# ACT's queue issues the first output-gate loads once both gate rows have landed

## What is computed

```python
for t in range(S):
    m_new = maximum(f_gate[:, :, t] + m, i_gate[:, :, t])
    f_stab, i_stab = exp(f_gate[:, :, t] + m - m_new), exp(i_gate[:, :, t] - m_new)
    m = m_new
    C = f_stab * C + i_stab * einsum('bhd,bhe->bhde', vt, kt)
    n = f_stab * n + i_stab * kt
    denom = maximum(abs(n . qt), 1.0)
    y[:, :, t] = sigmoid(o_gate[:, :, t]) * (C @ qt) / denom
x = y as (B, S, 320)
u = x + (relu(x^T @ w_tok1) @ w_tok2)^T
out = u + relu(u @ w_ch1) @ w_ch2
```

## Time and profile before

| | us |
|---|---|
| median of three runs | 469.45 (467.89 to 469.51) |
| time of the profiled execution | 467.59 |
| its span from the first to the last instruction | 465.9 |
| PE busy in the span | 442.2 (95%) |
| DVE busy | 264.2 |
| ACT busy | 228.9 |
| POOL busy | 176.8 |

### The profile page before, as it was taken

How to read it: one execution, slowest core, us unless ns; L and a number is a source line. 1 busy time by engine, 2 the same in 40 slices (tenths; PEclk the granted TensorE clock), 3 DMA queues, 4 the chain that set the end, 5 groups by cost and what they waited for, 6 DMA issues and landing times.

```text
span 465.9 us, 9523 instructions
## 1 busy us (share of the span) xinstructions
PE 442.2 (95%) x3471; PEld 408.0 (88%) x3471; DVE 264.2 (57%) x592; ACT 228.9 (49%) x570; POOL 176.8 (38%) x239
## 2 busy tenths in 40 slices
PE   6999989699999998999999998999999998999996
PEld 2577978589999997899999997899999997999996
DVE  6889964677766537666675227466685325222212
ACT  4665447657666247766653227966663113211111
POOL 6625410567665232676662203466663000000000
PEclk9999999999999999999999999999999999999999
DMA  7556990143444412444454012444410010000101
GB/s 210 195 156 185 348 267 30 37 123 118 138 135 153 135 46 86 138 139 138 127 161 127 13 42 85 135 128 137 139 59 1 2 42 1 0 2 0 44 1 42
DMA packets 36520, 47.38 MB, mean 102 GB/s; under 512 B 3324, under 2 KB 28986, under 8 KB 36474
## 3 DMA queue, kind: packets, MB, share of 16 engines
q1 hardware_dynamic: 35674, 45.79, 32.3%
q10 hardware_dynamic: 800, 0.98, 0.7%
HBM read 42.73 MB, written 4.03 MB: 100 GB/s over the span
## 4 chain that ended last, share of the span: by engine, by line
PE 80%; ACT 7%; DVE 5%; issue 4%; DMA 2%; SPq 1%; POOL 0%; DVEq 0%; ACTq 0%
PE pC L1155 31%; PE pA L1226 6%; PE pA L1227 6%; PE pA L1228 6%; PE pS L1067 6%; PE pA L1155 4%; PE pY L1124 4%; PE pA L1231 3%; PE pA L1230 3%; PE pY L1103 2%; PE pN L1079 2%; ACT gb L608 1%; PE pA L1185 1%; DMA u<-i_gate_dram 1%; DMA qz<-qT_dram 1%
## 5 line engine op out<-in xcount | busy, mean ns | idle before, releaser
L976 DVE SCALAR_TENSOR_TENSOR h_lo<-pA,h_hi 128x384 fp32r<-128x384 f32 x96 | 53.3, 555 | 133.1 <-ACT h_hi L758 133.1
L758 ACT ACTIVATE h_hi<-pA 128x384 fp32r<-128x384 f32 x96 | 46.7, 486 | 127.2 <-PE pA L1231 127.2
L1155 PE MATMUL pC<-wc_hi,h_hi 128*128 128x320 f32 x288 | 94.1, 327 | 0.8 <-DVE wc_lo L843 0.7
L1155 PE MATMUL pC<-wc_lo,h_hi 128*128 128x320 f32 x288 | 88.7, 308 | 0.0
L1155 PE MATMUL pC<-wc_hi,h_lo 128*128 128x320 f32 x288 | 88.4, 307 | 0.0
L490 POOL TENSOR_TENSOR gb<-gb,pb 128x384 f32<-128x384 f32 (+1 forms) x54 | 48.2, 893 | 81.9 <-ACT pb L618 81.9
L1226 PE MATMUL pA<-uT_hi,wc_hi 128*128 128x384 f32 x192 | 65.2, 340 | 1.9 <-DVE uT_hi L954 1.9
L1227 PE MATMUL pA<-uT_lo,wc_hi 128*128 128x384 f32 x192 | 64.7, 337 | 0.0
L1228 PE MATMUL pA<-uT_hi,wc_lo 128*128 128x384 f32 x192 | 64.4, 335 | 0.0
L1155 PEld LDWEIGHTS pC<-wc_hi,h_hi 128*128 128x128 f32 x288 | 54.0, 188 | 2.1 <-DVE h_lo L976 1.0
L1155 PEld LDWEIGHTS pC<-wc_lo,h_hi 128*128 128x128 f32 x288 | 54.2, 188 | 0.1
(11 more groups left out here) (128 smaller groups left out, 882.1 us busy)
## 6 DMA issues: line engine op xcount, KB each, us to landing
gb<-g_dram SPq DMA_DIRECT2D x18, 512.0 KB, 3.9
kv<-kvN_dram SPq DMA_DIRECT2D x24, 324.0 KB, 3.5
kd<-kT_dram SPq DMA_DIRECT2D x24, 180.0 KB
qz<-qT_dram SPq DMA_DIRECT2D x72, 60.0 KB
out_dram<-u SPq DMA_DIRECT2D x24, 160.0 KB, 1.9
qd<-qT_dram SPq DMA_DIRECT2D x20, 180.0 KB, 2.6
gq<-g_dram SPq DMA_DIRECT2D x45, 60.0 KB
wc_raw<-w_ch_dram SPq DMA_DIRECT2D x6, 384.0 KB, 5.3
```

The costliest lines, as they stand in the source:

```text
L758: nc.scalar.activation(h2[0][:, slot % 2], pA[slot % 2][:, 0:HALF], ACT.Relu).then_inc(h2_hi, 1)
L976: nc.vector.scalar_tensor_tensor(h2[1][:, slot % 2], pA[slot % 2][:, 0:HALF], 0.0, h2[0][:, slot % 2].bitcast(F32), ALU.max, ALU.subtract) ...
L1155: ins = mm(dst, a[p], b[q], start=first and n == 0, stop=last and n == 2)
```

## The change

ACT waits until both gate transfers have landed (`gates_in` at 32, the condition on which DVE's first scan waits too) before it issues its two loads of the first output gate. Nothing is removed and no transfer changes its size or its queue.

```diff
             o_tiles = o_gate[0, :, :].rearrange("(c p) d -> p c d", p=L)
+            act.wait_ge(gates_in, 32)
             for i, (first, last) in enumerate(O_PARTS):
                 act.dma_start(x[:, first:last], o_tiles[:, first:last]).then_inc(o_in[i], 16)
             sigmoid(0)
```

## The result

| | before | changed |
|---|---|---|
| median of six runs, us | 469.21 (467.89 to 469.51) | 472.62 (471.52 to 473.24) |
| profiled execution, us | 467.59 | 473.20 |
| span, us | 465.9 | 471.5 |

The changed kernel is slower: ratio 1.0077, 95% interval 1.0059 to 1.0094, that is 3.4 us. The forecast was +1.7, with a range that held the time; the sign was right and the size half. One execution of the changed kernel on the second chip took 1751.82 us, and nothing here shows why; no figure in this text counts it.

The account below looks back on a forecast made before the run. It took PE's nearly unbroken run from the query decays at 15.65 as the bound. Landing +2.6, waits -0.25 and -0.19, POOL slack -0.5 gave +1.7: 469.3 us profiled, 471.1 by the median; range 468.5 to 473.8.

Parts of the forecast that it names:

- The wait and the gates: Start of the kernel: the wait costs ACT at most 0.1 us; input gates land at 4.15, winning DVE 1.9 us.
- The third rival: Input gates still land near 6.1 because DMA engines are starting up; about +3.7 us; chance 0.07.
- The landing of the output gate: ACT's two loads, issued at about 4.2, land at 9.5, 2.6 us later than before, with ends 1.8 and 3.4.
- ACT's strand: On ACT, a fixed 4.79 us from landing to the end of `wT`; the 0.25 wait behind it goes.
- PE's gap and the clock: PE idles 3 to 4 us before spreading step 2 at about 15.2; whether its clock falls there was left open.
- The rival with a chance of 0.22: PE's clock falls in the new gap before step 2's spread, costing 1.8 more: about +3.5 us; chance 0.22.
- PE's wait for DVE: Before the query decays, PE's 0.19 us wait for DVE goes, since DVE's strand is done at 13.7.
- What is swallowed after: At segment 2's transposes, PE's 0.5 us wait for POOL absorbs part of the 2.16 shift, leaving +1.7.
- The rest of the chain moves along: After those transposes, later PE, DVE and SP steps shift with PE, at no cost and no gain.
- The sum: Whole kernel: +1.7 us, with a shift of 0.9 to 2.5 for the ends of the landing; chance 0.56.

Follow-up runs that it names:

- the repeat: The changed kernel itself run again, nothing edited, on a second chip: 471.87, 473.20 and 474.58 us, ratio 1.0112 against the kernel before.
- the identity's wait: Against the kernel before, ACT's two output-gate loads wait only until POOL has built the identity (1.54 us), not for the gates: 469.60 us, ratio 1.0047.

## Why the prediction was right in sign and short in size

- **The wait and the gates.** Right. The gates landed at 3.34, earlier than my 4.15 (issue to landing 2.09, not 2.9: their twin had been slowed by the output gate too). DVE was busy until 4.26 in any case, so the 1.9 won stood. The pieces of segment 1 came 2.6 earlier, at 13.00 and not 13.7, because one cast on the way (L814, now L815) took 0.59 and not 1.28; no run shows why, and nothing waited for it. The third rival, that they wouldn't come forward, is out.
- **The landing of the output gate.** This term was mis-sized: 4.1 later, where I took 2.6 and allowed 3.4. I had the issue at 4.2, and it was 3.37, which should have helped. What I had wrong was the length: 7.6 us, over my upper bound of 6.1, because I took today's pair as the worst case though today SP's loads move little beside it (the keys and values issued at 1.70 take 6.2 us to land before the change and 3.2 after it). SP's later loads cost 0.8 to 1.6 here. The Trainium skill ("DMA: Bandwidth & Descriptors", Rules for kernel authors) says to issue a DMA early and wait late. The 10.3 that the prediction made of it lies nearer to the 11.00 than my 9.5, but by luck: it rests on my late issue, and the same working from the measured 3.37 gives 9.5.
- **ACT's strand.** Right: from 11.00 to the start of the exponentials 4.73, against 5.04 before the change: the wait of 0.25 is gone, and 0.06 beside it.
- **PE's gap and the clock.** The rival with a chance of 0.22 is what happened, on top of a landing later than the rival had it. My gap of 3 to 4 us was 4.35, and PE's clock was at 0.50 from about 12.5. But the rival made the length of the gap the reason, and the clock fell when the gap was at most 0.7 us long. I had weighed against it that an idle of 2.13 had been harmless; the experiments show the clock falling around idles of 1.92 and 2.56, so the length of one gap says little either way. It costs 1.29 in the first profile and 2.3 in the second; my 1.8 was fair.
- **PE's wait for DVE.** I took off the 0.19 that the bracket gives. What went was 0.35 (2.75 against 2.40 from the spread to the query decays with the clock held), and with ACT's 0.31 the waits were worth 0.66, not 0.44.
- **What is swallowed after.** Wrong. I read 0.5 us of idle before the transposes of segment 2 as slack, since the profile names POOL as the releaser. In the changed kernel the same idle stands there, and its releaser is "issue" (first line before, second after):

```profile
23.41 0.13 PEld L1017 LDWEIGHTS pC<-ident,pb 32*128 32x128 f32 x1 [0.55 <-POOL u L482]
...
28.02 0.13 PEld L1018 LDWEIGHTS pC<-ident,pb 32*128 32x128 f32 x1 [0.55 <-issue]
```

  PE's scores before it start 4.61 later and the transposes 4.61 later. So nothing was waiting for POOL; it is idle time of the weight loads, which overlaps the matmul before, and the transposes of segment 1 have the same 0.55 with "issue" in both kernels. The 0.5 should not have been taken off.
- **The rest of the chain moves along.** Right: 4.71 at the query decays, 4.66 at the first matmul of the mixers.
- **The sum.** In the forecast's own terms: 4.08 (landing) - 0.66 (waits) + 1.29 (clock) - 0.05 = 4.66 at the mixers, where I had 2.6 - 0.44 - 0.5 = 1.7. So the forecast fell short by 1.5 in the landing, by 1.3 in the clock, which it left to a rival, and by 0.5 in the slack at POOL; its waits, 0.2 too small, went the other way. The 3.4 between the medians of the first chip is smaller than 4.66, and the 5.3 of the second is larger. Executions of one kernel differ by 2 us and more, and what brought the first medians closer than the profiles isn't shown.

## What to carry to other kernels

When several strands end at nearly the same moment, the chain names only one: ask for each of the others how late it is, because bringing the first forward gains no more than the distance to the second (0.66 us here, of 1.9). A transfer that is held back doesn't only start later, it meets whatever is issued meanwhile, and its length from an uncrowded moment is no upper bound. And fillers that keep TensorE's clock belong to a schedule: when a wait ends earlier or later, the gap moves away from them, and they are missing in the new gap and in the way at the old one.

## What the runs showed of the hardware that I had not expected

The granted clock fell to 0.50 near this gap in five traces, and not at a fixed distance from PE's idle time. In the changed kernel it fell at most 0.7 us after PE's last matmul. In the repeat it fell about 2 us after it (11.89, and between 13.80 and 14.30). With the keys and queries held back (an idle of 3.74), with the identity's wait (2.56) and with the input gates on ACT's queue (1.92) it fell 0.5 to 1.7 us after PE had begun again. The kernel before idles 2.13 ahead of its first transposes, and its five fillers behind them still took only 1.25. With fillers in the gap the clock held in all five traces that had them. What decides the moment no run here shows. In the column of the granted clock the slow beginning of the kernel (fillers 0.43 us apart) does not show, while the later falls do. And the two 96 KB loads of the gates landed 2.0 and 2.1 us after their issue once ACT's transfer no longer ran beside them, not 2.9 and 4.9:

```profile
u<-f_gate_dram SPq DMA_DIRECT2D x1, 96.0 KB, 2.0
u<-i_gate_dram SPq DMA_DIRECT2D x1, 96.0 KB, 2.1
```
